# Matmuls of ones in TensorE's waits at the start of a two-stage kernel

## The chip, the cores and the metric

The kernel runs on one core of one Trainium2 chip. The time is device microseconds of one execution; of several, the median is given. The engines are named TensorE (PE in the profile's rows, PEld for its weight loads), VectorE (DVE), ScalarE (ACT), GpSimd (POOL) and SyncE (SP), which here issues all transfers of data.

## What is computed

A recurrent attention and two gated feed-forward layers behind it, all in float32:

```python
for t in range(768):                       # batch 4, heads 8, head_dim 48
    kt, vt, rt = k[:, :, t], v[:, :, t], r[:, :, t]
    cur = einsum('bhd,bhe->bhde', u * kt, vt)
    y[:, :, t] = einsum('bhd,bhde->bhe', rt, state + cur)
    state = w * state + einsum('bhd,bhe->bhde', kt, vt)
x = y as [3072 tokens, 384]
x = (silu(x @ w_gate) * (x @ w_val)) @ w_out                 # 384 -> 1536 -> 384
xn = x / sqrt(mean(x * x) + 1e-6) * rms_g
out = (silu(xn @ w_gate2) * (xn @ w_val2)) @ w_out2
```

## The kernel before

The attention works on 24 chunks of 128 steps. In a chunk, pairs of steps up to 4 apart are summed on VectorE (`multiply_pairs`, `sum_pairs`: products with tables that GpSimd weighs in `weigh_k`, tile `pair_prod`), and pairs further apart come from TensorE in four levels (`level(g, l)`, 16 calls of 64x64 by 32 columns each, 32 records, line L903), whose operands VectorE and GpSimd scale with powers of w (`scale_r`, tile `r_level`; `scale_k`, tile `k_level`). The results go to `a_mat` by masked copies (`take_low`, `take_block` on VectorE, `take_third`, `take_high` on ScalarE). `sums(g)` (L919) sums the chunk's share of the state, which VectorE adds up in `sum_mid` and `sum_end`; `carried(g)` (L956) and `own(g)` (L973) make the chunk's output.

The first layer works on seven tiles of tokens, the first two of 2 chunks, the others of 4. A product of a layer is three float32r matmuls (`three_terms`, L810 to L812) over high and low parts of both operands. Every engine has one fixed order of work. In the first layer's tiles, the next chunks' attention is written into it by hand at slots (`LOW_AT`, `HIGH_AT`), and so is the splitting of weights: ScalarE copies the high part of a piece of 128x768 (`split_piece`), VectorE or GpSimd subtracts for the low part. Four pieces fit in `staging`; the load of piece 4 waits for the low part of piece 0, which VectorE makes. GpSimd also makes `h_lo`, the low part of every gated product, which TensorE's `down` group waits for.

The set-up ahead of this is what the change touches. Its order, engine by engine:

- TensorE: `level(0, 0..2)`, `turn_powers` (four transposes, L1086), `level(0, 3)`, `level(1, 0..2)`, `sums(0)`, `level(1, 3)`; for chunk 0 `carried`, `own`, `fill` (L988), for chunk 1 `sums`, `carried`, `own`, `fill`; then `begin_val` and the first groups of the first layer.
- VectorE: memsets, the table of powers with `scale_r(0, ..)`, `take_low(0)`, `scale_r(1, 0..2)`, `multiply_pairs` and `sum_pairs` of chunk 0, `take_block(0)`, `take_low(1)` (L1502), `sum_mid(0)` (L1572), `sum_end(0)`, `scale_r(1, 3)`, pairs of chunk 1, `sum_mid(1)` (L1575), `take_block(1)`, `sum_end(1)`, `first_lo(0)`, `split_piece(0)` (L1434), and so on.
- ScalarE: `take_third(0)`, `take_high(0)`, `pow_nat`, `split_piece(0)`, `take_third(1)`, `take_high(1)`, `split_piece(1)`, `copy_last(0)`, `copy_first(0)`, `split_piece(2)`, `copy_last(1)`, `copy_first(1)` (both wait for TensorE's chunk 1), `split_piece(3)`, `split_piece(4)` (tile `down_hi`, L1167).
- GpSimd: `scale_k(0, ..)`, a table, `weigh_k(0, 0)`, `scale_k(1, 0..2)`, `weigh_k(0, 1)`, `for_sums(0)` (waits for `pow_nat`), `scale_k(1, 3)`, `weigh_k(1, ..)`, `for_carried` and `for_sums`, `split_piece(1)`, `scale_k(2, ..)`, `split_piece(4)` (tile `down_lo`, L1833), `weigh_k(2, ..)`, then the first layer's `h_lo` (L1827) and the next chunks' work.
- SyncE: the tables and chunks 0 and 1, pieces 0 to 3, then loads that wait: chunk 2's for `y_done` of chunk 0, piece 4's for VectorE's `split_piece(0)`.

A float32 matmul that isn't float32r makes two records of TensorE, each with a weight load; a transpose and a float32r matmul make one. The second layer reads its tokens back from memory and works in two rounds of products; the change doesn't touch it. Its norm multiplies by ones (L1002), 128x512 in float32.

Of the kernel before, what the change touches and what calls it, by code (L numbers as in the profile page):

```python
# [14 lines left out]
P = 128  # L15
# [270 lines left out]

AHEAD = 2


def late_spot(g, part):  # L290

    return HIGH_AT[g] + int((LOW_AT[g + 1] - HIGH_AT[g]) * part)
# [55 lines left out]
def build(nc, a_t, a_n, r_blk, w_t, w_blk, w_last, weights, down2, blocks2, rms_g, level_mask, block_mask, turns, out,  # L348
          x2_dram, sums_dram):
    with ExitStack() as ctx:  # L350
# [10 lines left out]
        def sem(name):  # L361
            return ctx.enter_context(nc.semaphore(name))
# [27 lines left out]
        pow_up = sb("pow_up", [P, HP, HALF])  # L390
# [29 lines left out]
        def v_n(g):  # L420
            return chunk_in[:, g % 2, TW + DM:TW + NW].rearrange("p (h e) -> p h e", h=H)
# [67 lines left out]
        ps_val = ctx.enter_context(nc.psum_tensor("ps_val", [P, 2, BANK], F32))  # L489
        ps_down = ctx.enter_context(nc.psum_tensor("ps_down", [P, KT, BANK], F32))  # L490
        ps_level = ctx.enter_context(nc.psum_tensor("ps_level", [P, 2, BANK], F32))
# [35 lines left out]
            return a.rearrange("p (s h) t -> p s h t", s=2)  # L527

        w_in = sem("w_in")
        masks_in = sem("masks_in")  # L530
        turns_in = sem("turns_in")
        gain_in = sem("gain_in")
# [275 lines left out]
        def _(pe):  # L808
# [70 lines left out]
            def level(g, l):  # L879
                pe.wait_ge(r_scaled, LEVELS * g + l + 1)  # L880
                pe.wait_ge(k_scaled, LEVELS * g + l + 1)
                if l == 0:

                    if g > 1:
                        pe.wait_ge(high_in, g)
                        sums_taken(pe, g - 1)
                elif l == FIRST_TWO and g >= SIZES[0]:

                    pe.wait_ge(low_in, FIRST_TWO * (g + 1))
                elif l == LOW and g < SIZES[0]:  # L890
                    pe.wait_ge(low_in, FIRST_TWO * (g + 1))
                    pe.wait_ge(third_in, g + 1)
                for hp in range(HP):
                    for c in range(2):
                        for slot in range(2):
                            rows = slice(slot * SLOT, (slot + 1) * SLOT)
                            if l < LOW:
                                left = k_low[rows, l, hp, c * HALF:(c + 1) * HALF]
                            else:

                                at = LOW * HP * CH + hp * HALF + c * 32
                                left = k_level[rows, at:at + HALF]
                            last = nc.tensor.matmul(level_out(g, l)[c * HALF:(c + 1) * HALF, slot, hp, :], left,  # L903
                                                    r_level[rows, l, hp, c * 32:c * 32 + 32], start=True, stop=True)
                last.then_inc(level_done, 1)

            def sums(g):


                pe.wait_ge(kv_loaded[g % 2], 16 * (g // 2 + 1))  # L910
                pe.wait_ge(k_state_done, g + 1)
                if g < SIZES[0]:
                    pe.wait_ge(high_in, g + 1)
                for hp in range(HP):
                    for slot in range(2):
                        for half in range(1 if g % CPB == CPB - 1 else 2):
                            rows = slice(half * HALF, (half + 1) * HALF)
                            place = slot * HP + hp
                            last = nc.tensor.matmul(sums_out(g, half)[slot * SLOT:slot * SLOT + D, hp, :], k_state[rows, place, :],  # L919
                                                    v_n(g)[rows, place, :], start=True, stop=True)  # L920
                last.then_inc(sums_done, 1)
# [3 lines left out]
            def carried(g, turn):  # L925

                if turn == 0:
                    pe.wait_ge(block_in, g + 1)  # L930
                    pe.wait_ge(r_state_done, g + 1)
                    if g + 1 < NCH and g != 1:

                        pe.wait_ge(r_scaled, LEVELS * (g + 2))
                    if g == 1:
                        pe.wait_ge(mid_done, g + 1)
                    else:
                        sums_taken(pe, g)
                    if g >= SIZES[0]:
                        reach(pe, y_copied, g)  # L940
                    else:
                        pe.wait_ge(state_zero, 3)
                else:
                    pe.wait_ge(y_begun, g + 1)
                width = SLOT if g < SIZES[0] else D
                for n in range(2):
                    for side in range(2):
                        for slot in range(2):
                            half = slot if turn else 1 - slot
                            if half == 0 and g and g % CPB == 0:  # L950
                                continue
                            hp = 2 * side + n
                            rows = slice(slot * SLOT, slot * SLOT + D)
                            before = state_mid_of(g)[rows, hp, 0:width] if half else state_in[rows, g % 2, hp, 0:width]
                            at = (slot * 2 + n) * HALF
                            last = nc.tensor.matmul(result_out(g, half)[side * SLOT:side * SLOT + width, at:at + HALF], before,  # L956
                                                    r_state_of(g)[rows, hp, half * HALF:(half + 1) * HALF],
                                                    start=(g, side, half) not in begun, stop=False, skip_group_check=True)
                            begun.add((g, side, half))
                if turn == 0:  # L960
                    last.then_inc(y_begun, 1)

            def own(g):

                pe.wait_ge(kv_loaded[g % 2], 16 * (g // 2 + 1))
                for slot in range(2):
                    for n in range(2):
                        for side in range(2):
                            for half in range(2):
                                rows = slice(half * HALF, (half + 1) * HALF)  # L970
                                place = slot * HP + 2 * side + n
                                at = (slot * 2 + n) * HALF
                                last = nc.tensor.matmul(result_out(g, half)[side * SLOT:side * SLOT + D, at:at + HALF],  # L973
                                                        v_n(g)[rows, place, :], a_of(g)[rows, place, :],
                                                        start=(g, side, half) not in begun, stop=True, skip_group_check=True)
                                begun.add((g, side, half))
                last.then_inc(y_done, 1)

            def fill(g):

                pe.wait_ge(turns_in, 16)
                pe.wait_ge(last_copied, g + 1)
                for kt in range(KT):
                    for half in range(2):
                        for side in range(2):
                            rows = slice(side * SLOT, (side + 1) * SLOT)
                            c = g * CH + half * HALF
                            last = nc.tensor.matmul(result_out(g, half)[rows, kt * HALF:(kt + 1) * HALF], select[rows, kt, rows],  # L988
                                                    y_last[rows, c:c + HALF], start=False, stop=True, skip_group_check=True)
                last.then_inc(y_filled, 1)  # L990
# [91 lines left out]
            def turn_powers():  # L1082
                pe.wait_ge(pow_reversed, 1)
                pe.wait_ge(turns_in, 16)
                for hp in range(HP):
                    last = nc.tensor.transpose(ps_gate[:, hp * P:(hp + 1) * P], pow_turn[:, hp, :], ident)  # L1086
                last.then_inc(pow_turned, 1)

            for l in range(LOW):
                level(0, l)  # L1090
            turn_powers()
            level(0, LOW)
            for l in range(LOW):
                level(1, l)
            sums(0)
            level(1, LOW)
            for g in range(SIZES[0]):
                if g:
                    sums(g)
                carried(g, 0)  # L1100
                carried(g, 1)
                own(g)
                fill(g)
            pe.wait_ge(pow_nat_done, 1)
            begin_val()
            for t in range(TILES1):
# [316 lines left out]
        def _(dve):  # L1423
# [264 lines left out]
                dve.wait_ge(table_step, count[0])  # L1688


            nc.vector.memset(pow_up[:, :, 0:1], 1.0)
            chain(nc.vector.memset(pow_near[:, :, 0:1], 1.0))
            nc.vector.memset(a_mat[:], 0.0).then_inc(a_mat_zero, 1)
            nc.vector.memset(state_in[:], 0.0).then_inc(state_zero, 1)
# [407 lines left out]
```

## Time and profile before

| | |
|---|---|
| median of 3 runs | 997.6 us (996.66 to 997.73) |
| the profiled execution | 996.6 us |
| its span, first to last instruction | 994.7 us |
| TensorE busy | 959.1 us, 96% of the span |
| VectorE, ScalarE, GpSimd busy | 704.7, 401.8, 565.5 us |

The profile is that of one execution. Times of rows count from the span's start. A matmul's record is longer than its share of TensorE, as matmuls overlap: the spacing of the starts tells the pace. "<-" behind idle time names what ended it; "issue" is idle time for which the profile shows no such thing.

### The profile page before, as it was taken

The page shows a single profiled execution, that of the slowest core. Times are in us where ns is not written, and L with a number is a line of the kernel's source. Part 1 is how long each engine was busy: PE and PEld are TensorE (multiplying, and loading weights), DVE is VectorE, ACT ScalarE, POOL GpSimd, SP SyncE. Part 2 cuts the span into 40 slices and gives each one's busy share as a digit, 9 for nine tenths or more (in the row PEclk, how much of TensorE's full clock was granted, in tenths as well). Part 3 has the DMA queues.
Part 4 walks back from the last instruction along what each step waited for, and adds up shares of the span by engine and source line. Part 5 has one row for each costly group of instructions (what it writes and reads, how often), then busy time and mean ns, then how long its engine had stood idle before and what let it go on. Part 6 is the DMA issues. An engine that isn't in the chain of part 4 may idle for free.

```text
span 994.7 us, 23699 instructions
## 1 busy us (share of the span) xinstructions
PE 959.1 (96%) x9324; PEld 794.8 (80%) x9324; DVE 704.7 (71%) x1123; ACT 401.8 (40%) x839; POOL 565.5 (57%) x446
## 2 busy tenths in 40 slices
PE   4898999999999999999999999999999999999998
PEld 4898997888888888888877777787888777878876
DVE  7888677576857756675429968788677899567760
ACT  3463334334333433433432454434633436344423
POOL 8898986556666666466233325678526787211134
PEclk9999999999999999999999999999999999999999
DMA  6663443535434343543142156443064441254201
GB/s 256 217 216 112 141 148 115 176 116 176 176 130 149 130 149 108 179 151 110 64 154 85 42 182 222 159 149 116 33 220 152 147 159 54 102 174 159 80 0 64
DMA packets 50348, 136.06 MB, mean 137 GB/s; under 512 B 6656, under 2 KB 9664, under 8 KB 50240
## 3 DMA queue, kind: packets, MB, share of 16 engines
q1 hardware_dynamic: 50240, 134.56, 38.5%
q8 instruction: 75, 1.23, 0.5%
q14 instruction: 33, 0.27, 0.1%
HBM read 108.29 MB, written 25.17 MB: 134 GB/s over the span
## 4 chain that ended last, share of the span: by engine, by line
PE 73%; POOL 9%; DVE 8%; issue 7%; DMA 2%; ACT 1%; POOLq 0%; SPq 0%; DVEq 0%; ACTq 0%
PE ps_down L810 7%; PE ps_down L812 6%; PE ps_down L811 6%; PE ps_val L810 6%; PE ps_val L811 5%; PE ps_val L812 5%; PE ps_gate L810 5%; PE ps_gate L812 5%; PE ps_gate L811 5%; PE ps_level L903 4%; PE ps_level L1056 2%; PE ps_level L1058 2%; PE ps_level L1057 2%; PE ps_val L956 1%; PE ps_val L1056 1%
## 5 line engine op out<-in xcount | busy, mean ns | idle before, releaser
L1827 POOL TENSOR_TENSOR h_lo<-h_raw,h_hi 128x512 fp32r<-128x512 f32 (+1 forms) x84 | 114.8, 1367 | 203.1 <-ACT h_hi L1162 194.3
L810 PE MATMUL ps_down<-h_hi,down_hi 128*128 128x512 f32 (+1 forms) x360 | 134.9, 375 | 0.9 <-DVE room_c L1671 0.9
L812 PE MATMUL ps_down<-h_lo,down_hi 128*128 128x512 f32 (+1 forms) x360 | 132.6, 368 | 0.0
L811 PE MATMUL ps_down<-h_hi,down_lo 128*128 128x512 f32 (+1 forms) x360 | 132.6, 368 | 0.0
L1162 ACT ACTIVATE h_hi<-h_raw 128x512 fp32r<-128x512 f32 (+1 forms) x84 | 47.9, 571 | 153.5 <-DVE h_raw L1428 153.4
L1428 DVE TENSOR_TENSOR h_raw<-h_raw,ps_val 128x512 f32<-128x512 f32 (+1 forms) x84 | 51.1, 608 | 82.9 <-PE ps_val L812 75.0
L810 PE MATMUL ps_gate<-x_hi,up_weights 128*128 128x512 f32 (+1 forms) x252 | 93.9, 373 | 2.2 <-ACT h_raw L1156 1.3
L810 PE MATMUL ps_val<-x_hi,up_weights 128*128 128x512 f32 (+1 forms) x249 | 90.9, 365 | 5.2 <-DVE h_raw L1428 3.3
L812 PE MATMUL ps_gate<-x_lo,up_weights 128*128 128x512 f32 (+1 forms) x252 | 91.0, 361 | 0.3 <-issue 0.3
L1870 POOL TENSOR_TENSOR pair_prod<-chunk_in,w_block 128x768 f32<-128x768 f32 x47 | 91.3, 1943 | 0.0
L811 PE MATMUL ps_gate<-x_hi,up_weights 128*128 128x512 f32 (+1 forms) x252 | 90.9, 361 | 0.0
L811 PE MATMUL ps_val<-x_hi,up_weights 128*128 128x512 f32 (+1 forms) x249 | 89.6, 360 | 0.0
L812 PE MATMUL ps_val<-x_lo,up_weights 128*128 128x512 f32 (+1 forms) x249 | 89.5, 360 | 0.0
L1156 ACT ACTIVATE h_raw<-ps_gate 128x512 f32<-128x512 f32 (+1 forms) x84 | 45.1, 537 | 97.4 <-PE ps_gate L812 95.5
L1858 POOL TENSOR_TENSOR k_level<-chunk_in,pow_up 128x256 f32<-128x256 f32 x96 | 79.4, 838 | 3.8 <-DMA chunk_in<-in_a_t_dram 3.4
L1845 POOL TENSOR_TENSOR h_lo<-h_second,h_hi 128x512 fp32r<-128x512 f32 x36 | 50.4, 1400 | 51.8 <-ACT h_hi L1316 51.7
L810 PEld LDWEIGHTS ps_down<-h_hi,down_hi 128*128 128x128 f32 x360 | 67.8, 188 | 13.7 <-issue 1.7
L812 PEld LDWEIGHTS ps_down<-h_lo,down_hi 128*128 128x128 f32 x360 | 67.8, 188 | 11.5
L811 PEld LDWEIGHTS ps_down<-h_hi,down_lo 128*128 128x128 f32 x360 | 67.9, 188 | 10.9
L1056 PE MATMUL ps_level<-x_sum_hi,ring 128*128 128x512 f32 x162 | 64.4, 397 | 1.8 <-DVE h_second L1671 0.8
L1057 PE MATMUL ps_level<-x_sum_hi,ring 128*128 128x512 f32 x162 | 63.2, 390 | 0.0
L1058 PE MATMUL ps_level<-x_sum_lo,ring 128*128 128x512 f32 x162 | 63.1, 390 | 0.0
(293 smaller groups left out, 2456.5 us busy)
## 6 DMA issues: line engine op xcount, KB each, us to landing
ring<-sums_dram SPq DMA_DIRECT2D x72, 640.0 KB, 4.8
r_block<-in_r_blk_dram SPq DMA_DIRECT2D x24, 768.0 KB, 4.9
chunk_in<-in_a_t_dram SPq DMA_DIRECT2D x24, 512.0 KB, 3.6
chunk_in<-in_a_n_dram SPq DMA_DIRECT2D x24, 384.0 KB, 4.4
sums_dram<-sum_lo SPq DMA_DIRECT2D x24, 320.0 KB, 3.0
staging<-in_weights_dram SPq DMA_DIRECT2D x18, 384.0 KB, 4.0
raw<-in_blocks_dram SPq DMA_DIRECT2D x8, 576.0 KB, 5.4
sums_dram<-sum_hi SPq DMA_DIRECT2D x12, 320.0 KB, 2.4
```

Of the source, the lines that this page charges most:

```text
L810: nc.tensor.matmul(dst, w_hi, x_h, start=first, stop=False)
L811: nc.tensor.matmul(dst, w_lo, x_h, start=False, stop=False)
L812: return nc.tensor.matmul(dst, w_hi, x_l, start=False, stop=last)
L1056: nc.tensor.matmul(place, hi, x_h, start=p == chain[0], stop=False, skip_group_check=True)
L1057: nc.tensor.matmul(place, lo, x_h, start=False, stop=False, skip_group_check=True)
L1058: nc.tensor.matmul(place, hi, x_l, start=False, stop=True, skip_group_check=True).then_inc(step_done, 1)
L1162: nc.scalar.activation(h_hi[:, f % 3, 0:WIDTH[t]], h_raw[:, f % 2, 0:WIDTH[t]], ACT.Copy).then_inc(h_hi_done, 1)
L1428: nc.vector.tensor_tensor(h_raw[:, f % 2, 0:WIDTH[t]], h_raw[:, f % 2, 0:WIDTH[t]], ps_val[:, 0, 0:WIDTH[t]], ALU.mult)\
L1827: nc.gpsimd.tensor_tensor(h_lo[:, f % 3, 0:WIDTH[t]], h_raw[:, f % 2, 0:WIDTH[t]], h_hi[:, f % 3, 0:WIDTH[t]].bitcast(F32), ALU.subtract). ...
L1845: nc.gpsimd.tensor_tensor(h_lo[:, u % 3, :], h_of(r, q, 2 * m + n), h_hi[:, u % 3, :].bitcast(F32), ALU.subtract)\
L1858: nc.gpsimd.tensor_tensor(place, k_t(g).rearrange("p h (b x l) -> p h b x l", x=2, l=L)[:, :, :, 0, :], pow_up[:, :, L - 1::-1].unsqueeze( ...
L1870: nc.gpsimd.tensor_tensor(pair_prod[:, part, :], k_n(g).unsqueeze(1).broadcast_to([P, BLK // 2, DM]), w_block[:, part, :], ALU.mult).then_ ...
```

## The change

TensorE gets a function `keep_up(n, place)`: n matmuls of a 128x128 operand of ones with itself (column 0 of `pow_up`, broadcast), float32, into a place of PSUM that nobody reads (`spare`, in `ps_val`, or `spare_later`, in `ps_level`). It is called at the start, behind a wait for VectorE's memset of that column (semaphore `one_in`), and behind the steps of the set-up, 61 matmuls in all. Nothing else is changed.

```diff
+UP_FIRST, UP_LEVELS, UP_TURNED, UP_UPPER, UP_SECOND, UP_SUMS = 11, (1, 1, 3), 4, 3, (3, 1, 5), 14
+UP_RESULT, UP_OWN, UP_FILLED = (2, 5), (4, 2), (0, 2)
...
+            def keep_up(n, place):
+                for _ in range(n):
+                    nc.tensor.matmul(place, pow_up[:, 0, 0:1].broadcast_to([P, P]), pow_up[:, 0, 0:1].broadcast_to([P, P]),
+                                     start=True, stop=True, skip_group_check=True)
+
+            spare, spare_later = ps_val[:, 0, 0:P], ps_level[:, 1, 0:P]
+            pe.wait_ge(one_in, 1)
+            keep_up(UP_FIRST, spare)
             for l in range(LOW):
                 level(0, l)
+                keep_up(UP_LEVELS[l], spare)
             turn_powers()
+            keep_up(UP_TURNED, spare)
             level(0, LOW)
+            keep_up(UP_UPPER, spare)
             for l in range(LOW):
                 level(1, l)
+                keep_up(UP_SECOND[l], spare)
             sums(0)
+            keep_up(UP_SUMS, spare)
             level(1, LOW)
             for g in range(SIZES[0]):
                 if g:
                     sums(g)
+                keep_up(UP_RESULT[g], (spare, spare_later)[g])
                 carried(g, 0)
                 carried(g, 1)
                 own(g)
+                keep_up(UP_OWN[g], spare_later)
                 fill(g)
+                keep_up(UP_FILLED[g], spare_later)
...
-            nc.vector.memset(pow_up[:, :, 0:1], 1.0)
+            nc.vector.memset(pow_up[:, :, 0:1], 1.0).then_inc(one_in, 1)
```

## Rows read from the trace of the kernel before

**Rows 1.** The page: TensorE's part of the busy times, and TensorE's queue of instructions.

```profile
PE 959.1 (96%) x9324; PEld 794.8 (80%) x9324; DVE 704.7 (71%) x1123; ACT 401.8 (40%) x839; POOL 565.5 (57%) x446
...
q8 instruction: 75, 1.23, 0.5%
```

**Rows 2.** Windows: busy us of each engine, granted clock, DMA share, GB/s.

```profile
0.00:35.20 35.20, 19.61 (x506) 17.49 (x507) 27.75 (x65) 11.71 (x28) 26.77 (x26) 1.00 0.71 261
35.20:93.80 58.60, 54.91 (x1065) 52.25 (x1064) 49.84 (x71) 26.76 (x63) 58.24 (x43) 1.00 0.49 167
93.80:994.70 900.90, 884.56 (x7755) 725.03 (x7755) 627.14 (x988) 363.30 (x749) 480.48 (x377) 1.00 0.37 130
```

**Rows 3.** TensorE's timeline, 5 to 40 us: start, us, instruction, idle time before.

```profile
5.90 2.85 PE L903 MATMUL ps_level<-r_level,k_level 64*64 64x32 f32 x96 [5.90 <-POOL k_level L1858]
9.35 1.09 PE L1086 MATMUL ps_gate<-x_raw 128*128 128x128 f32 x4 [0.60 <-DMA x_raw<-in_turns_dram]
11.07 1.08 PE L903 MATMUL ps_level<-r_level,k_level 64*64 64x32 f32 x32 [0.63 <-ACT a_mat L1236]
12.54 1.08 PE L903 MATMUL ps_down<-r_level,k_level 64*64 64x32 f32 x32 [0.39 <-POOL k_level L1858]
14.01 1.72 PE L903 MATMUL ps_down<-r_level,k_level 64*64 64x32 f32 x55 [0.39 <-POOL k_level L1858]
18.47 0.53 PE L903 MATMUL ps_down<-r_level,k_level 64*64 64x32 f32 x9 [2.75 <-issue]
18.71 0.96 PE L919 MATMUL ps_level<-chunk_in,k_state 64*48 64x48 f32 x32
21.35 1.08 PE L903 MATMUL ps_down<-r_level,k_level 64*64 64x32 f32 x32 [1.69 <-DVE r_level L1489]
...
35.35 0.41 PE L810 MATMUL ps_gate<-x_hi,up_weights 128*128 128x256 f32 x1
35.56 0.41 PE L811 MATMUL ps_gate<-x_hi,up_weights 128*128 128x256 f32 x1
...
39.65 0.28 PE L810 MATMUL ps_gate<-x_hi,up_weights 128*128 128x256 f32 x1
39.77 0.28 PE L811 MATMUL ps_gate<-x_hi,up_weights 128*128 128x256 f32 x1
```

**Rows 4.** TensorE's instruction queue, 15.5 to 16.5 us; a window; SyncE's issues.

```profile
q8 instruction: 1, 0.02, 6.9%
...
10.00:12.00 2.00, 1.37 (x35) 1.00 (x33) 1.08 (x3) 0.89 (x4) 2.00 (x3) 1.00 1.00 416
...
6.19 1.93 SPq L663 DMA_DIRECT2D staging<-in_weights_dram  x4
```

**Rows 5.** VectorE's timeline, 19 to 30 us.

```profile
19.03 0.43 DVE L1502 COPY_PREDICATED a_mat<-masks,ps_down 128x256 f32<-128x256 int32 x1 [0.23 <-PE ps_down L903]
19.84 0.35 DVE L1572 COPY state_mid<-ps_level 128x192 f32<-128x192 f32 x1
...
27.60 0.35 DVE L1575 TENSOR_TENSOR x_out<-x_out,ps_down 128x192 f32<-128x192 f32 x1 [0.26 <-PE ps_down L919]
...
29.67 0.95 DVE L1434 TENSOR_TENSOR up_weights<-staging,up_weights 128x768 fp32r<-128x768 f32 x1
```

**Rows 6.** ScalarE's timeline at 34 us.

```profile
34.31 0.84 ACT L1167 ACTIVATE down_hi<-staging 128x768 fp32r<-128x768 f32 x1
```

**Rows 7.** GpSimd's timeline, 35 to 44 us.

```profile
35.23 2.64 POOL L1833 TENSOR_TENSOR down_lo<-staging,down_hi 128x768 fp32r<-128x768 f32 x1 [3.34 <-ACT down_hi L1167]
...
43.13 1.15 POOL L1827 TENSOR_TENSOR h_lo<-h_raw,h_hi 128x256 fp32r<-128x256 f32 x1 [0.27 <-ACT h_hi L1162]
```

**Rows 8.** SyncE's issue of pieces 4 and 5, and piece 4's time to landing.

```profile
30.71 0.81 SPq L663 DMA_DIRECT2D staging<-in_weights_dram  x2
...
DMA to landing us min/median/max: 3.2/3.2/3.2
```

**Rows 9.** TensorE's timeline at 516 us: the norm, one call, two records.

```profile
516.56 1.02 PE L1002 MATMUL ps_level<-norm_room,ones 128*128 128x512 f32 x2
```

## What the change was forecast to do

> **What bounds the kernel now.** I read the windows of three stretches first. Behind 93.8 us TensorE is busy for 884.56 of 900.90 us; between 35.2 and 93.8 us GpSimd is busy for 58.24 of 58.60 us and TensorE for 54.91 [rows 2]. So the second stretch belongs to GpSimd, whose order of work is fixed, and the long third stretch only starts later or earlier as the second lets it. The extra matmuls all lie in the first 35 us. The question is therefore not how fast TensorE gets there, but when GpSimd's unbroken run begins and what the change does to it.
>
> GpSimd's run begins with `down_lo` at 35.23 us, after an idle time of 3.34 us that ScalarE's `down_hi` ended; behind it GpSimd waits once more, for 0.27 us [rows 7]. `down_hi` is copied at 34.31 us [rows 6] out of a piece whose load SyncE issued at 30.71 us and which took 3.2 us, so it landed at 33.9 us [rows 8]. That load waits for VectorE's `split_piece(0)` (29.67 to 30.62 us), the end of a VectorE queue that since 19.03 us has idled for just one 0.26 us, waiting for `sums(1)` [rows 5]. So VectorE sets GpSimd's start, with 0.4 us (33.9 to 34.31) in which ScalarE's place behind TensorE's fill counts.
>
> Next TensorE's timeline. It waits, as the change supposes, and it runs slowly: 256-column matmuls start 0.21 us apart at 35.35 us and 0.12 us apart from 39.65 us on [rows 3]. The column of the granted clock says 1.00 in all three stretches [rows 2] and doesn't show this; by the spacing, 256 columns in 0.21 us are 1.2 GHz, and later the full 2.4 GHz. By the spacing the engine rose only at about 39.3 us, after its first unbroken full-width work.
>
> The view that decided me is one gap in it. After 55 of the 64 records that follow 14.01 us TensorE stands still from 15.73 to 18.47 us, and the profile knows nobody it waits for ("issue" 2.75) [rows 3]. Until there it has run 96 + 4 + 32 + 32 + 55 = 219 matmuls and as many weight loads: 438 instructions. The queue of instructions moved 75 packets in the whole run, for 18,648 matmuls and weight loads, 249 to a packet [rows 1], and its first packet since the start lies between 15.5 and 16.5 us [rows 4]. I read this as a fetch of code. TensorE had used up what it held and stood until the next block came. If a block is asked for when one packet's worth is still in hand, the asking was at instruction 438 - 249 = 189, the end of the third level at about 8.6 us. It came 7 us later, presumably behind data: 416 GB/s at 10 us, and four staging loads issued from 6.19 us on [rows 4].
>
> **The change, part by part.**
>
> *The price of one.* A matmul of ones is float32, 128 columns, and makes two records with a weight load each, as the norm's two records show (one call). Slow, four full-width 128-column records took 1.09 us from first to last end at 9.35 us [rows 3]: 0.21 us apart, so 0.43 us for one. Fast, two 512-column records take 1.02 us with their tail, 0.43 us apart [rows 9]; a quarter of that would be 0.11 us, and 0.12 us is the closest that full-width pairs run here [rows 3]: 0.24 us for one. There are 61: 26 us slow, 15 us fast. Nothing is removed; VectorE's memset gains a semaphore, no time.
>
> *The first 11.* From about 0.95 us, 11 x 0.43 = 4.7 us, to 5.65 us. The first level starts at 5.90 us [rows 3]: no cost.
>
> *Behind the three levels, the transposes and the upper level (1, 1, 3, 4, 3).* Fast, they fit: the next step waits for GpSimd or a load. Slow, 12 x 0.43 us push `pow_nat` and with it GpSimd by 1 to 2 us; GpSimd has 3.34 us to give there [rows 7]. Zero for the end.
>
> *What they do to the code.* Each one is four instructions. By the start of `level(1, 1)` the stream holds 11 x 4 = 44, three levels 192, five 20, transposes 8, four 16, `level(0, 3)` 64, three 12, `level(1, 0)` 64, three 12: 432. So the 438th falls three records into `level(1, 1)`, at about 14.0 us, where before it fell 55 records later. Number 189 is reached at about 7.6 us, a microsecond earlier, with at least three of the four staging loads ahead of it; one load is 384 KB, 0.9 us at 416 GB/s. So the block comes at best 0.9 us sooner: TensorE resumes between 17.5 and 18.5 us. I take 18.0.
>
> *Behind the resumption.* Before, 9 records and `sums(0)` were left, over at 19.67 us. Now 61 records of levels are left (1.65 us at 0.027 each: the 55 took 1.72 us, of which one record's own 0.28 us is tail), then 1 and 5 matmuls of ones, then `sums(0)` (0.96 us). With the slow clock after 3 to 4 us of standing: 18.0 + 1.65 + 6 x 0.43 + 0.96 = 23.2 us. VectorE's `sum_mid(0)`, at 19.84 us, waits for it: +3.5 us. Behind it are queued all of VectorE's pair products for chunk 1, its `take_block(1)` and `split_piece(0)` [rows 5]; no idle time behind can absorb it but 0.26 us. The 14 ones then run 3.4 us if the rate has risen and 6.0 us if not. With a few slow ones, `level(1, 3)` comes near 27.5 us instead of 21.35, and with its ones, carried, own, fill and `sums(1)` TensorE is at about 32 us where VectorE, itself 3.5 us late, wants it at 31.1: up to 1 us more. VectorE's `split_piece(0)` thus ends 3.2 to 4.2 us late, the piece lands at 37.1 to 38.1 us, ScalarE takes 0.8 us, and GpSimd starts at 38.0 to 39.0 us instead of 35.23. Less the 0.27 us wait: +2.5 to +3.5 us. A second fetch, falling behind the chunk loads that follow `y_done(0)`, may hold `fill(1)`; I put 0.3 us on it for its chance, and keep 3 us for the bound.
>
> *The gain.* If the rate is up by chunk 1's `carried`, the matmuls from 35.35 us on save 0.09 us each, 1.6 us for eighteen, and carried, own and fill some 2 us more. All of it lies ahead of matmuls that wait for GpSimd's `h_lo`. To the end it gives nothing.
>
> *Sum.* +3.0 (middle) + 0.3 = +3.3 us on 996.6 us, the profiled execution's own time (span 994.7): 999.9. The median of the runs is 997.6, 1.0 above, so 1000.9 us.
>
> The Trainium skill's Runtime: NRT & Kernel Launch (Instruction fetch mechanics) has code refilled in blocks of 256 instructions, gives TensorE room for 2,048, and calls a crossing mostly hidden. The block size agrees with the 249 above; the room and the hiding don't agree with a stop at 438. By that page the sum would lack the stop, which is rival 2.
>
> **Rivals.**
>
> 1. *The stop comes, but TensorE resumes fast.* Then 61 records take about 1.2 us, six ones 1.4, `sums(0)` 0.6: 21.2 us, VectorE +1.4, GpSimd +1 to +1.8. Time 998.6 to 999.4. For it: 4.7 us of full-width work at the start, nearly unbroken to 14 us. Against: the standing of 3.5 to 4.5 us, and the slow spacing that still stood at 35.56 us, half-busy set-up or not [rows 2, 3]. [...]
> 2. *No stop, or elsewhere without harm.* Then VectorE loses its waits of 0.23 and 0.26 us [rows 5], and ScalarE its 0.4 us: GpSimd starts at most 0.9 us sooner, with its own 0.27 us 1.1. Time 996.5 to 997.6. For it: an earlier request may slip between loads. Against: the 7 us that it took.
> 3. *Faster.* GpSimd's run isn't the bound and TensorE's gains (2 + 1.6 us) arrive: 994 to 995.5. Place: `h_lo` of the first tile. It decides if GpSimd shows waits above 2 us between 35 and 94 us; before it shows 0.27 [rows 7]. Its single operations may change pace, too, with what the other engines do beside them.
> 4. *The rate never rises before 39 us.* The 14 cost 6.0 us and all behind stays slow: sums(1) near 36 us, +6 us or more: 1003 and up.
>
> **How the numbers follow.** Forecast 0.45, rivals 0.2, 0.2, 0.1, 0.05. 0.2% is 2 us, about what the three runs can tell. The forecast's case reaches from +2 to +6 us; nearly all of it is slower by over 0.2%, as is rival 4 and a bit of rival 1: slower 0.52. Rivals 1 and 2 are within: same 0.35. Rival 3 and a corner of 2: faster 0.13. The range leaves out rival 3 and most of rival 4: low 996.4 (rival 2's end), high 1004.2 (the forecast with the second fetch in full). The slower case alone would be 999.6 to 1003.6.
>
> **What would show it.** Right: an "issue" gap of TensorE that starts near 14 us with three records of `level(1, 1)` done, ended at 17.5 to 18.5 us; `sum_mid(0)` of VectorE at 23 us; `down_lo` of GpSimd at 38 to 39 us, no wait above 0.3 us behind it until 94 us; there the records of before, all shifted alike. Wrong: no gap (rival 2), 0.24 us per matmul of ones right behind 18 us (rival 1), or a shift of GpSimd that the end doesn't share (rival 3). What would undo it most simply is a block of code that arrives in time.

## The result, and the profile after

| | before | changed |
|---|---|---|
| median | 997.66 us (22 runs, 995.89 to 999.62) | 1000.45 us (22 runs, 996.31 to 1005.76) |
| ratio, 95% interval | | 1.0027 (1.0017 to 1.0038) |
| profiled execution, span | 996.6, 994.7 us | 1000.64, 998.8 us |

The change costs 2.8 us. First the page of the changed kernel and its windows, the stretches cut 4.1 us later than in [rows 2].

```profile
PE 972.4 (97%) x9446; PEld 807.2 (81%) x9446; DVE 704.1 (70%) x1123; ACT 401.9 (40%) x839; POOL 561.8 (56%) x446
...
q8 instruction: 76, 1.25, 0.5%
...
0.00:39.30 39.30, 35.42 (x680) 32.02 (x683) 29.40 (x66) 11.50 (x28) 25.22 (x26) 0.91 0.63 232
39.30:98.00 58.70, 52.65 (x1026) 50.34 (x1019) 47.05 (x69) 27.37 (x64) 55.84 (x43) 0.97 0.49 168
98.00:998.80 900.80, 884.32 (x7755) 724.86 (x7755) 627.61 (x988) 363.02 (x749) 480.73 (x377) 1.00 0.38 130
```

The third stretch is that of before (900.80 against 900.90 us, the same 7,755 matmuls): the loss lies ahead of it. TensorE got 122 more records (61 x 2) and is busy for 35.42 us instead of 19.61 in the first stretch, so the change does what it says. Its timeline answers to [rows 3].

```profile
0.92 5.06 PE L1097 MATMUL ps_val<-pow_up 128*128 128x128 f32 x22 [0.92 <-DVE pow_up L1713]
...
12.76 0.67 PE L907 MATMUL ps_down<-r_level,k_level 64*64 64x32 f32 x32
...
15.24 0.67 PE L907 MATMUL ps_down<-r_level,k_level 64*64 64x32 f32 x32
...
17.65 3.39 PE L1097 MATMUL ps_val<-pow_up 128*128 128x128 f32 x28
23.46 0.92 PE L907 MATMUL ps_down<-r_level,k_level 64*64 64x32 f32 x32 [2.42 <-DVE r_level L1511]
24.31 1.22 PE L1097 MATMUL ps_val<-pow_up 128*128 128x128 f32 x4
...
27.75 2.07 PE L1097 MATMUL ps_level<-pow_up 128*128 128x128 f32 x8
29.75 1.20 PE L992 MATMUL ps_val<-y_last,x_raw 64*64 64x64 f32 x22
...
30.81 0.55 PE L923 MATMUL ps_down<-chunk_in,k_state 64*48 64x48 f32 x30
...
46.53 0.36 PE L814 MATMUL ps_val<-x_hi,up_weights 128*128 128x256 f32 x1 [3.08 <-DVE h_raw L1450]
```

No gap with "issue" stands in it: the 2.75 us of [rows 3] at 18.47 are gone, and TensorE runs through to 21.04 us. The levels behind the first ones take 0.67 us instead of 1.08. Then it stands for 2.42 us, waiting for VectorE, and is slow again: 8 records of ones take 2.07 us at 27.75 us, where 28 took 3.39 at 17.65 us. Windows of it (wall time, busy times as in [rows 2], granted clock third from the end):

```profile
21.00:23.40 2.40, 0.04 (x1) 0.00 (x0) 2.30 (x8) 1.07 (x4) 2.40 (x2) 1.00 0.72 289
...
28.00:30.00 2.00, 2.00 (x12) 1.77 (x14) 0.59 (x2) 0.22 (x2) 1.01 (x1) 0.50 0.51 123
30.00:32.00 2.00, 2.00 (x62) 1.95 (x61) 0.56 (x2) 0.95 (x3) 0.56 (x1) 0.87 1.04 404
```

The granted clock is 0.50 (1.2 GHz) at 28 us, behind that standing. The column knows only what the trace's clock records hold. In this kernel the first record begins at 6.64 us, in before at 38.27 us, both with the full clock; ahead of them the column prints 1.00 though nothing is recorded. So the 1.00 of [rows 2] is no reading of the clock up to 38.27 us. Now VectorE, for [rows 5].

```profile
13.41 1.27 DVE L1548 TENSOR_TENSOR pair_prod<-pair_prod,r_block 128x768 f32<-128x768 f32 x1 [1.71 <-DMA r_block<-in_r_blk_dram]
...
21.95 0.35 DVE L1594 COPY state_mid<-ps_level 128x192 f32<-128x192 f32 x1
...
31.45 0.35 DVE L1597 TENSOR_TENSOR x_out<-x_out,ps_down 128x192 f32<-128x192 f32 x1 [2.85 <-PE ps_down L923]
...
33.51 1.42 DVE L1456 TENSOR_TENSOR up_weights<-staging,up_weights 128x768 fp32r<-128x768 f32 x1
```

`sum_mid(0)` is 2.11 us late and does not wait for TensorE. The lateness begins at the first product, which waits 1.71 us for `r_block`. Two rows of before that were not shown yet, the same product and the end of GpSimd's run:

```profile
12.32 0.96 DVE L1526 TENSOR_TENSOR pair_prod<-pair_prod,r_block 128x768 f32<-128x768 f32 x1 [0.76 <-DMA r_block<-in_r_blk_dram]
...
96.92 0.94 POOL L1827 TENSOR_TENSOR h_lo<-h_raw,h_hi 128x256 fp32r<-128x256 f32 x1 [3.19 <-ACT h_hi L1162]
```

The wait has grown by 0.95 us. `x_out` then waits 2.85 us for `sums(1)`, where it waited 0.26 [rows 5]; it is 3.85 us late, `split_piece(0)` 3.84, and that takes 1.42 us instead of 0.95. SyncE, ScalarE and GpSimd follow, for [rows 6 to 8]:

```profile
35.02 0.81 SPq L667 DMA_DIRECT2D staging<-in_weights_dram  x2
...
38.79 0.84 ACT L1189 ACTIVATE down_hi<-staging 128x768 fp32r<-128x768 f32 x1 [1.91 <-DMA staging<-in_weights_dram]
...
39.71 1.85 POOL L1855 TENSOR_TENSOR down_lo<-staging,down_hi 128x768 fp32r<-128x768 f32 x1 [5.59 <-ACT down_hi L1189]
...
100.83 0.94 POOL L1849 TENSOR_TENSOR h_lo<-h_raw,h_hi 128x256 fp32r<-128x256 f32 x1 [3.17 <-ACT h_hi L1184]
```

GpSimd's `down_lo` is 4.48 us late, the `h_lo` at the end of its run 3.91, with nearly the same wait ahead of it, and the span is 4.1 us longer.

Where does the first wait come from? In before, the queue of instructions moved nothing from the start to 15 us [rows 4]. Here its first packet lies in the window from 11 to 12 us:

```profile
q8 instruction: 1, 0.02, 5.5%
...
r_block<-in_r_blk_dram SPq DMA_DIRECT2D x1, 768.0 KB, 8.1
```

The share is of 16 engines: one packet held one engine for 0.055 x 16 x 1 us = 0.9 us. The second line is the load of `r_block` that SyncE issued at 5.27 us: landed after 8.1 us. In before it took 7.1.

### The profile page after: what moved, and what is told of

Read it like the earlier page. It is cut to its first block, busy times and chain, and to the rows that moved or that the text cites. A ratio compares the mean times of both kernels' runs of the same rounds, so it can differ in the third digit from the quotient of the medians.

```text
span 998.8 us, 23943 instructions
## 1 busy us (share of the span) xinstructions
PE 972.4 (97%) x9446; PEld 807.2 (81%) x9446; DVE 704.1 (70%) x1123; ACT 401.9 (40%) x839; POOL 561.8 (56%) x446
## 4 chain that ended last, share of the span: by engine, by line
PE 73%; DVE 8%; issue 7%; POOL 6%; DMA 3%; ACT 2%; SPq 1%; POOLq 0%; DVEq 0%; ACTq 0%
PE ps_down L814 7%; PE ps_down L815 6%; PE ps_down L816 6%; PE ps_val L814 6%; PE ps_val L816 6%; PE ps_val L815 6%; PE ps_gate L814 5%; PE ps_gate L816 5%; PE ps_gate L815 5%; PE ps_level L907 4%; PE ps_level L1060 2%; PE ps_level L1062 2%; PE ps_level L1061 2%; PE ps_val L960 1%; PE ps_val L1060 1%
## 5 line engine op out<-in xcount | busy, mean ns | idle before, releaser
L1880 POOL TENSOR_TENSOR k_level<-chunk_in,pow_up 128x256 f32<-128x256 f32 x96 | 76.5, 809 | 5.6 <-DMA chunk_in<-in_a_t_dram 5.3
```

The lines of the kernel that those rows point to most:

```text
L1880: nc.gpsimd.tensor_tensor(place, k_t(g).rearrange("p h (b x l) -> p h b x l", x=2, l=L)[:, :, :, 0, :], pow_up[:, :, L - 1::-1].unsqueeze( ...
```

## The experiments

They stand in the order in which they were run: the first four together, then the next four, then the last four. The two theories after the result were that the early packet of code delays `r_block`, and that the six ones ahead of `sums(1)` delay `sums(1)` and VectorE behind it; the forecast's own (TensorE stands for code, and VectorE for TensorE) was their rival. Theory D, formed behind the first four, is that added instructions move the places where blocks of code end. Each ratio is to the kernel before, with its 95% interval.

**Only the ones ahead of `level(1, 0)`** (23 stay; the expectation says 20).

```diff
-... UP_UPPER, UP_SECOND, UP_SUMS = 11, (1, 1, 3), 4, 3, (3, 1, 5), 14
-UP_RESULT, UP_OWN, UP_FILLED = (2, 5), (4, 2), (0, 2)
+... UP_UPPER, UP_SECOND, UP_SUMS = 11, (1, 1, 3), 4, 3, (0, 0, 0), 0
+UP_RESULT, UP_OWN, UP_FILLED = (0, 0), (0, 0), (0, 0)
```

> Only the 20 matmuls of ones ahead of level(1, 0) stay; the other 41 are left out. Theory A (the loss is made late: the six ones between level(1, 3) and the fill of chunk 0 stand in front of sums(1), at half clock): sums(1) near 27 us, VectorE waits under 0.5 us for it, GpSimd's down_lo within 1.2 us of 35.2 us, time within 0.1% of before. Theory B (the loss is made early: code and load traffic move, r_block of chunk 0 lands 1 us later and VectorE is late from 13 us on): VectorE starts the first product at 13.4 us again, down_lo at 36.5 us or later, time 1.001 to 1.002 of before. Theory C, the prediction's (TensorE stands for code and all behind is late): an issue gap of TensorE at a number of instructions near 440.

1000.72 us (8 runs), 1.0034 (1.0022 to 1.0045).

```profile
13.65 1.06 DVE L1548 TENSOR_TENSOR pair_prod<-pair_prod,r_block 128x768 f32<-128x768 f32 x1 [1.95 <-DMA r_block<-in_r_blk_dram]
...
37.11 2.65 POOL L1855 TENSOR_TENSOR down_lo<-staging,down_hi 128x768 fp32r<-128x768 f32 x1 [3.33 <-ACT down_hi L1189]
...
62.78 0.43 PE L977 MATMUL ps_val<-a_mat,chunk_in 64*48 64x64 f32 x14 [1.81 <-issue]
```

The early ones alone bring the packet at 11 to 12 us, `r_block` after 8.3 us, and `down_lo` 1.88 us late. That is what the first theory expects. The loss of the run isn't explained by it: TensorE stands for code at places where before had nothing, 62.78 us (1.81), 110.10 (0.50) and 331.19 (1.43). Theory D comes from here.

**Without the six ones ahead of `fill(0)` and `sums(1)`** (55 stay).

```diff
-UP_RESULT, UP_OWN, UP_FILLED = (2, 5), (4, 2), (0, 2)
+UP_RESULT, UP_OWN, UP_FILLED = (0, 5), (0, 2), (0, 2)
```

> The change without the 2 ones behind level(1, 3) and the 4 between own and fill of chunk 0 (55 stay). Theory A: sums(1) comes 2.5 to 3 us sooner than in the changed kernel, VectorE's wait of 2.85 us falls below 0.5 us, down_lo at 36.5 to 37.5 us instead of 39.7, time 0.9975 of the changed kernel's, about 1.0005 of before. Theory B: that wait is only a symptom; down_lo stays above 38.5 us and the time at 1.002 to 1.003 of before.

999.88 us (12 runs), 1.0021 (1.001 to 1.0032).

```profile
29.34 0.35 DVE L1597 TENSOR_TENSOR x_out<-x_out,ps_down 128x192 f32<-128x192 f32 x1 [0.16 <-PE ps_down L923]
...
37.15 2.31 POOL L1855 TENSOR_TENSOR down_lo<-staging,down_hi 128x768 fp32r<-128x768 f32 x1 [3.53 <-ACT down_hi L1189]
```

The wait of 2.85 us is 0.16, and `down_lo` is 1.92 us late instead of 4.48: the second theory is shown in the profile. (In the other profile of this kernel, the last run, the wait is 0.87 us.) The time missed the expectation of 1.0005. In the medians the six are hard to see, so the pair ran again beside each other (last).

**Only the ones behind the second group's result, own and fill** (15 stay).

```diff
-... = 11, (1, 1, 3), 4, 3, (3, 1, 5), 14
+... = 0, (0, 0, 0), 0, 0, (0, 0, 0), 0
```

> Only the late 15 ones stay, around carried, own and fill of both chunks; the 46 ahead of level(1, 3) are left out, so that TensorE never is at the full clock there. Theory A: each costs 0.43 us, six of them 2.6 us in front of sums(1): VectorE waits 2 to 2.5 us, down_lo at 37.5 to 38.5 us, time 1.002 to 1.003 of before. Theory B: no early ones, no loss: 0.9995 to 1.0005 of before.

1001.91 us (7 runs), 1.0041 (1.0024 to 1.0058). With nothing early, the packet falls in 16 to 17 us, `r_block` takes 7.1 us and the product waits 0.77, as in before; the code stop is back (18.60, 3.03 us). `sums(1)` is waited for 2.77 us, `down_lo` starts at 37.47. The second theory is there alone. Again TensorE stands for code later, 1.82 us at 62.81 and 1.69 at 242.08.

**All 61, but tiny** (4 columns by 32 rows of output instead of 128 by 128).

```diff
-nc.tensor.matmul(place, pow_up[:, 0, 0:1].broadcast_to([P, P]), pow_up[:, 0, 0:1].broadcast_to([P, P]),
+nc.tensor.matmul(place[0:32, 0:4], pow_up[:, 0, 0:1].broadcast_to([P, 32]), pow_up[:, 0, 0:1].broadcast_to([P, 4]),
```

> All 61 stay but as matmuls of 32x4 instead of 128x128: as many instructions, almost no time in TensorE, and hardly any activity. Theory A: no loss, down_lo within 1 us of 35.2 us, time 0.999 to 1.0005 of before. Theory B (code traffic does it): the first product of VectorE at 13.4 us and a time 1.001 to 1.002 of before. Theory C: TensorE stands near its 440th instruction, at 13 to 18 us, and VectorE's copy behind sums(0) comes 1 to 2 us later than in before.

1000.0 us (11 runs), 1.0027 (1.0016 to 1.0037): with their work nearly all gone, the 244 instructions cost as much as the ones. But this isn't the change with its work alone taken out: the levels take 1.08 us again, as in before, and the first clock record, with the full clock, begins at 42.43 us. The packet comes at 11 to 12 us, `r_block` after 8.4, `down_lo` at 37.71 (`sums(1)` is waited for 1.34 us instead of 2.85); TensorE stands for code 1.33 us at 419.64.

**The two kernels once more**, unedited, one execution each, to see what of the profile repeats.

> The kernel before, unchanged, for a second profile. If the place of the first code packet goes with the order of the instructions and not with chance: packet near 16 us, VectorE's first product of chunk 0 at 12.3 us, the issue gap of 2.75 us behind the same 55 records, GpSimd's down_lo at 35.2 us.

> The changed kernel, unchanged, for a second profile. Packet near 11.3 us and the first product at 13.4 to 14.0 us, as in all four kernels with early ones. Open is the clock: if the fall to half at 24 us is a matter of chance, the six ones in front of sums(1) cost 1.4 us here instead of 3, and VectorE waits about 1.3 us for sums(1) instead of 2.85.

Before: 997.28 us, span 995.4. Changed: 1001.88, span 1000.0. Two lines of before, then three of the changed kernel:

```profile
13.43 1.36 DVE L1526 TENSOR_TENSOR pair_prod<-pair_prod,r_block 128x768 f32<-128x768 f32 x1 [0.92 <-DMA r_block<-in_r_blk_dram]
...
19.41 0.53 PE L903 MATMUL ps_down<-r_level,k_level 64*64 64x32 f32 x9 [3.03 <-issue]
```

```profile
14.12 1.78 DVE L1548 TENSOR_TENSOR pair_prod<-pair_prod,r_block 128x768 f32<-128x768 f32 x1 [1.76 <-DMA r_block<-in_r_blk_dram]
...
32.16 0.35 DVE L1597 TENSOR_TENSOR x_out<-x_out,ps_down 128x192 f32<-128x192 f32 x1 [2.86 <-PE ps_down L923]
...
41.32 1.84 POOL L1855 TENSOR_TENSOR down_lo<-staging,down_hi 128x768 fp32r<-128x768 f32 x1 [6.43 <-ACT down_hi L1189]
```

The stop, with the same 9 records behind it, and the two waits repeat. The start itself does not: this execution of before has VectorE and GpSimd 0.8 to 1.4 us later than the first, and its span is only 0.7 longer. So I read the waits and the time to landing, not the clock times alone.

**Six tiny ones at the start, and nothing else**: 24 instructions with almost no work.

```diff
-... UP_UPPER, UP_SECOND, UP_SUMS = 11, (1, 1, 3), 4, 3, (3, 1, 5), 14
+... UP_UPPER, UP_SECOND, UP_SUMS = 6, (0, 0, 0), 0, 0, (0, 0, 0), 0
...
+nc.tensor.matmul(place[0:32, 0:4], pow_up[:, 0, 0:1].broadcast_to([P, 32]), pow_up[:, 0, 0:1].broadcast_to([P, 4]),
```

> Before, plus six matmuls of 32x4 at 0.9 us, in a wait of 4 us: 24 instructions and nothing else; the 61 ones are left out. Theory B, sharpened (the early code packet shares the queues with r_block of chunk 0, whose last part then lands over 1 us late, and VectorE with it): the packet moves from 16 to about 11.3 us, VectorE's first product from 12.3 to 13.5 us, down_lo to 36.3 to 37.3 us, time 1.001 to 1.0025 of before, and the issue gap at 15.7 us is gone. Rival: 24 instructions do nothing, 1.000 of before, and the loss comes from the time and the clock of the ones.

1001.09 us (6 runs), 1.004 (1.0026 to 1.0054): slower by as much as all 61, and not by `r_block` (waited for 0.77 us; the packet came at 14 to 15 us and not at 11.3, behind the landing). TensorE stands for code at the last record of a tile's `own`, GpSimd, at the end of its run, waits 5.10 us where it waited 3.19, and the granted clock is 0.50 from 99.0 to 102.4 us:

```profile
96.72 0.21 PE L977 MATMUL ps_val<-a_mat,chunk_in 64*48 64x64 f32 x1 [1.83 <-issue]
...
100.17 0.93 POOL L1849 TENSOR_TENSOR h_lo<-h_raw,h_hi 128x256 fp32r<-128x256 f32 x1 [5.10 <-ACT h_hi L1184]
...
99.00:102.40 3.40, 3.40 (x18) 3.40 (x17) 1.85 (x4) 0.80 (x2) 2.23 (x3) 0.50 0.63 235
```

**Only the middle ones** (`UP_SECOND` and `UP_SUMS`, 23). This restores the code ahead of the stop, so it is the test of the forecast's own mechanism.

```diff
-... = 11, (1, 1, 3), 4, 3, (3, 1, 5), 14
-UP_RESULT, UP_OWN, UP_FILLED = (2, 5), (4, 2), (0, 2)
+... = 0, (0, 0, 0), 0, 0, (3, 1, 5), 14
+UP_RESULT, UP_OWN, UP_FILLED = (0, 0), (0, 0), (0, 0)
```

> Only the 23 ones behind level(1, 0..2) and sums(0) stay; ahead of them the code is that of before. Theory C, the prediction's, in the place where its condition is kept (same packet near 16 us): TensorE stands with 15 records of level(1, 2) done, until 18.4 us; then 17 records, five slow ones and sums(0) end near 22 us, VectorE's copy behind it at 22.2 instead of 19.8 us, the 14 ones take up to 6 us, sums(1) comes after 31 us and the time is 1.003 to 1.006 of before; r_block lands as in before (first product at 12.3 us). Theory B alone: no early code, so 1.000 to 1.001.

1001.27 us (8 runs), 1.0037 (1.0023 to 1.005).

```profile
18.08 0.65 PE L907 MATMUL ps_down<-r_level,k_level 64*64 64x32 f32 x15
19.71 0.74 PE L907 MATMUL ps_down<-r_level,k_level 64*64 64x32 f32 x17 [0.98 <-issue]
...
23.77 0.36 DVE L1594 COPY state_mid<-ps_level 128x192 f32<-128x192 f32 x1 [2.36 <-PE ps_level L923]
...
39.17 1.82 POOL L1855 TENSOR_TENSOR down_lo<-staging,down_hi 128x768 fp32r<-128x768 f32 x1 [2.90 <-ACT down_hi L1189]
...
63.62 0.43 PE L977 MATMUL ps_val<-a_mat,chunk_in 64*48 64x64 f32 x14 [1.41 <-issue]
```

TensorE stops after 96 + 4 + 32 + 32 + 6 + 32 + 2 + 15 = 219 records, the very number of before, now 17 records short of the level's end. `sum_mid(0)` waits 2.36 us for it, and `down_lo` is 3.94 us late (2.51 against the second execution of before, whose start is as late as this one's): the forecast's chain. The late gap stands at the same 14 records as with the early ones only. Both add 92 instructions, at different places ahead of it.

**Six, then twelve tiny ones behind `sums(0)`, and nothing else**: 24 instructions at another place, and 48, for the question whether place or count sets the gap.

```diff
-... UP_UPPER, UP_SECOND, UP_SUMS = 6, (0, 0, 0), 0, 0, (0, 0, 0), 0
+... UP_UPPER, UP_SECOND, UP_SUMS = 0, (0, 0, 0), 0, 0, (0, 0, 0), 6     # second kernel: 12
```

> Before, plus the same six matmuls of 32x4 as in the run with six at the start, but behind sums(0), in TensorE's wait of 1.7 us at 19.7 us; the 61 ones are left out. Theory D (all later code is shifted by 24 instructions, and a block boundary falls where TensorE runs through small matmuls faster than code comes): an issue gap of about 1.8 us at the own() records near 96 us, as in the run with six at the start, with nothing else changed: time 1.0015 to 1.003 of before. Theory B (only the early place of the first packet costs): 1.000 of before, no such gap.

> The same with twelve tiny ones, a shift of 48 instructions, 1.4 us of a wait of 1.7 us. Theory D: the gaps change place, and none is at the own() records near 96 us; by the shift of 92, which had three gaps of 0.5 to 1.8 us, and of 24, which had one, I expect one or two, 1.001 to 1.004 of before. If only the number of added instructions counted and not their remainder, the loss would be twice that of six.

Six: 1003.47 us (6 runs), 1.0049 (1.003 to 1.0068). Twelve: 1001.68 (12 runs), 1.0034 (1.0024 to 1.0044). The gap in the one and in the other:

```profile
98.06 0.21 PE L977 MATMUL ps_val<-a_mat,chunk_in 64*48 64x64 f32 x1 [1.71 <-issue]
```

```profile
95.33 0.43 PE L977 MATMUL ps_val<-a_mat,chunk_in 64*48 64x64 f32 x13 [1.99 <-issue]
```

Six at either place put the gap one record ahead of the end of `own`; 24 instructions more put it 12 records (24 instructions) sooner, 13 ahead of the end. I had expected no gap near 96 us for the twelve: the place moved with the count instead of going away. Count, not place, sets it.

The other profiles say the same. Counted from TensorE's first record, the "issue" gaps of 0.45 us and more stand behind 219, 721, 963 or 964, 1,580, 1,829, 2,454, 2,582, 3,950 or 3,951, 5,199 and 6,448 records, in whichever kernel they come; most of these numbers recur in two kernels or more, and the steps from the first to the others are close to multiples of 124.6 records, 249 instructions. And each of these gaps ends 1.2 to 1.6 us behind the end of a packet of TensorE's queue: in before the packet runs from 15.98 to 17.09 us, and TensorE resumes at 18.47. One "issue" gap does neither, 0.96 us ahead of `sums(0)` in the run of the early ones alone: it ends as GpSimd's `k_state` is done.

In the profile of the six there is more: piece 4's load, issued at 32.33 us, had a code packet beside it at 34 to 35 us, and `down_hi` began 5.52 us behind the issue (3.60 in before). What these three kernels lose in the median (0.40, 0.49 and 0.34% of 997.7 are 4.0, 4.9 and 3.4 us) is more than a gap of 1.7 to 2.0. Part of the rest is the clock: in both profiles of six tiny ones it is at 0.50 from 99.0 to 102.4 and from 99.3 to 102.7 us, behind the gap. The profile of the twelve has the gap of 1.99 us and no such fall; its span is 1.8 us longer than that of before, and it is the fastest of the twelve executions (998.32 to 1003.78). The remainder isn't settled.

**The changed kernel and the one without the six ones, beside each other**, unedited from above.

> The changed kernel once more, beside the next one. Half clock from about 24 us, VectorE's wait of 2.8 us for sums(1) as in both profiles so far; 1.0025 to 1.004 of before.

> The change without the six ones in front of chunk 0's fill, beside the changed kernel. If the six cost what the profiles say (down_lo 2.6 us sooner), 1 to 2.5 us faster than the changed kernel; if GpSimd or the code takes it back, under 0.7 us, as the medians of separate runs had it (0.6 us).

Changed: 1000.08 us (12 runs), 1.0018 (1.0005 to 1.0031), `down_lo` at 38.78. Without the six: 998.74 us (12 runs), 1.0004 (0.9993 to 1.0015), `down_lo` at 36.88. The medians differ by 1.3 us; with twelve executions each that isn't clear of noise (resampled, the difference lies between -0.6 and +3.0). What is shown of the six is their 1.9 us of GpSimd's start.

The profiled execution without the six also shows what a late gap can cost beside itself:

```profile
419.47 0.46 PE L977 MATMUL ps_val<-a_mat,chunk_in 64*48 64x64 f32 x6 [1.65 <-issue]
...
419.50:422.90 3.40, 3.40 (x13) 2.68 (x14) 2.13 (x7) 2.13 (x5) 0.00 (x0) 0.50 0.52 168
```

Behind the standing of 1.65 us the granted clock is 0.50, and 512-column matmuls start 0.43 us apart instead of 0.23. From the end of GpSimd's run (98.10 us) this execution takes 901.9 us, 4.1 more than the 897.8 of before. With the 61 tiny ones the gap at the same record is 1.33 us, the clock stays at 1.00, and the same stretch takes 899.2 us, 1.4 more.

## Why the prediction was right, and where it was not

1. **The bound** was right. GpSimd's start at 35.23 us sets the rest. Its delay of 4.48 us makes the span 4.1 us longer; without the six ones, with no large gap behind, 1.92 us make 2.2. TensorE's own gain didn't arrive, as forecast: at 46.53 us it waits 3.08 us for VectorE's `h_raw`.
2. **The stop.** "So the block comes at best 0.9 us sooner" is the step that failed. It came 4.75 us sooner (11.23 us against 15.98), ahead of its need at 14 us, and the stop was gone. In all seven profiles of kernels that kept the 11 first matmuls, tiny or not, the packet falls in 11 to 12 us; in the seven without them, between 14 and 18. The count of records to the stop was exact, and with the same code ahead the forecast's chain came in kind: with the middle ones alone VectorE waits 2.36 us for TensorE, where the forecast had 3.5. (The stop moved by 52 records, not 55: the 55 count from the start of `level(1, 1)`.) My number 189 for the asking, with the loads ahead of it as a nearly fixed delay, was only argued, and the traces speak against it. TensorE began its 95th record, instruction 189, at 8.45 us in before and at 8.39 us in the changed kernel (not at 7.6, as forecast), and the packets began 7.5 and 2.8 us behind that. When a packet is asked for stays open.
3. **What took its place.** Rival 2 had "no stop", and then 0 to -1.1 us. The stop went, the gain didn't come. First, `r_block` came late. In the seven profiles with the early packet the first product waits 1.71 to 2.32 us for it, in the seven without 0.76 to 0.92, with no overlap. The load took 8.1 to 8.8 us with the early packet and 7.1 without, where SyncE issued it at 5.2 to 5.4 us; in four executions without it, issued at 5.7 to 5.9 us, it took 7.7 to 8.1. That the packet makes the delay, by taking a turn on the loads' engines, is argued and not shown: no kernel moved the packet alone, and the six tiny ones at the start, meant to, moved it only to 14.56 us. VectorE, which sets GpSimd's start, was late from its first product on; `sum_mid(0)` was forecast 3.5 us late because of TensorE, and came 2.11 late without waiting for it. Its second product with `r_block`, now beside GpSimd's weighing, took 2.44 us instead of 1.63, which is part of the 2.11.
4. **The rate.** The price of one was right: 28 records in 3.39 us are 0.24 us for one, 22 in 5.06 us 0.46, and 8 in 2.07 us 0.52 with their tail. The forecast had the six ahead of `sums(0)` slow. They were fast, and the six ahead of `sums(1)` were slow, behind a standing of 2.42 us that VectorE's lateness made. "Up to 1 us more" was the term for them; the wait grew by 2.59 us. This is the term that was mis-sized.
5. **The load of piece 4** was taken as unchanged. From its issue to `down_hi` it is 3.77 us in the profile above, with a code packet at 35 to 36 us, 4.61 us in the second profile of the same kernel, with one at 36 to 37 us, and 3.02 us in the third, with none from 33 to 41 us. The link isn't shown: without the six ones the load took 3.8 us to land with no packet beside it, and with the early ones alone 3.1 us with one.
6. **The sum.** Forecast 1000.9 us, measured 1000.45, by another way. In the profiled execution VectorE is 1.26 us late where it begins to wait for `sums(1)` (31.45 - 2.85 = 28.60, before 27.60 - 0.26 = 27.34), the wait adds 2.59, a longer `split_piece(0)` 0.46 and the load 0.17: 4.48 us. The forecast had 3.0 by the moved stop. That the numbers meet is chance: the medians lose 2.8 us, less than this one profile.
7. **Missing:** the ends of the other blocks of code. Added instructions shift them all, and kernels with 15 to 23 of the ones, or 6 tiny ones, were no faster than the full change, in good part, by argument, for that reason: their profiles hold 1.8 to 3.7 us of such gaps behind 40 us. The 244 instructions of the change hit no gap above 0.74 us behind 40 us in the first profile, and one of 1.31 us at 43.60 in another. Missing, too, was the clock behind such a standing. In the 22 executions of the changed kernel the time goes with the mean granted clock: the four at 1.000 took 996.3 to 999.9 us, the other 18 took 998.6 to 1005.8, and the two lowest, 0.993 and 0.991, took 1003.2 and 1005.8. Which of the two brings the other isn't shown, and the mean hides a late first rise: the tiny 61, at half pace up to 42 us, read 1.000 too.

The Trainium skill's Runtime: NRT & Kernel Launch (Instruction fetch mechanics) calls the crossing of a block mostly hidden. Most of the 76 are. The stops of 2.75 and 3.03 us, and the gaps of 1.3 to 2.0, are not.

## What to carry to other kernels

Work that fills a wait is not free where the engine is fed from memory: count its instructions, see where the blocks of code then come relative to the loads that the path waits for, and look for "issue" gaps in and behind bursts of small matmuls far from the edit, and for a lower granted clock behind them. Fill only to where the wait ends: 0.5 us for a matmul at half clock, ahead of the step that the next engine needs, delays it; six of them here were 2.0 to 2.7 us of VectorE's wait. For an edit of 0.3%, run the same instructions with no work in them beside it, and check that its clock rises at the same place; here that version cost the same, but its clock rose 36 us later.

## What the runs showed of the hardware

- One 16 KB packet of code took one of 16 engines for 0.9 us while the loads ran. Where it fell at 11 to 12 us, VectorE waited 1.71 to 2.32 us for the 768 KB load in flight, else 0.76 to 0.92 us (seven profiles each).
- TensorE stood for code 2.75 and 3.03 us in two executions of before, both after 219 records. Later gaps of 1.3 to 2.0 us stood in bursts of small matmuls or up to 17 full-width records behind one, and moved by 12 records for 24 instructions. The same kernel can show one or not: without the six ones, 1.65 us at 419.47 in one profile, none above 0.40 in the other. That such a gap is a block fetched late is inferred, since the profile names nobody for it; but all of 0.45 us and more, save the one that ends with `k_state`, stood at block ends by count, and TensorE resumed 1.2 to 1.6 us behind the end of a packet.
- 24 instructions of almost no work cost 0.4 and 0.5% (1.0026 to 1.0054 and 1.003 to 1.0068).
- Full-width matmuls ran at half pace up to 39 us in before [rows 3]; the trace's first clock record, with the full clock, begins at 38.27 us, and the 1.00 in [rows 2] ahead of it stands for no record. In the changed kernel the full pace was there from 6.9 us on, and 0.50 was granted behind a standing of 2.42 us. Behind a gap of 1.65 us at 419.47 it was 0.50 up to 422.9 us; behind one of 1.33 us at 419.64 it stayed 1.00.

Open: why starts differ by a microsecond between executions; what beside the gap and the clock behind it the tiny ones cost; whether the early packet itself delays `r_block`. Not tried: loads ordered so that the early packet meets none that the path needs, and padding that moves all block ends out of the bursts. No kernel here was faster than the one before.
